# Moving two small tensors and dropping an unused one in a fused attention and MoE kernel

## The reference

```python
# attention (linear, with decay w and bonus u); r, k, v: (4, 8, 768, 48)
for t in range(S):
    cur = einsum('bhd,bhe->bhde', u * k[t], v[t])
    y[t] = einsum('bhd,bhde->bhe', r[t], state + cur)
    state = w * state + einsum('bhd,bhe->bhde', k[t], v[t])
x = y as (3072 tokens, 384)
# first layer, d_ff = 768
h = maximum(maximum(x @ w1, x @ w2), x @ w3);  x = h @ w_out
# second layer, d_ff = 1536
xn = x / sqrt(mean(x * x) + 1e-6) * rms_g
out = (silu(xn @ w_gate) * (xn @ w_val)) @ w_out
```

## Time and profile before

| | |
|---|---|
| median of 3 runs | 918.44 us (918.18 to 918.67) |
| the profiled execution | 918.18 us |
| its span | 916.3 us |
| TensorE matmuls busy | 878.3 us (96%) |
| VectorE, ScalarE, GpSimd busy | 428.6, 318.6, 157.2 us |
| mean granted TensorE clock | 0.989 |

### The profile page before, as it was taken

The page is one execution under the profiler, slowest core; times in us unless marked ns, Lnnn a source line. Parts: engine busy times, 40 slices in busy tenths (PEclk is TensorE's granted clock), DMA queues, the critical chain, the costliest instruction groups (busy, mean ns, idle before and its releaser), DMA issues.

```text
span 916.3 us, 13898 instructions
## 1 busy us (share of the span) xinstructions
PE 878.3 (96%) x4776; PEld 796.2 (87%) x4776; DVE 428.6 (47%) x985; ACT 318.6 (35%) x716; POOL 157.2 (17%) x197
## 2 busy tenths in 40 slices
PE   3689999999999999999989999999999999999998
PEld 3579999999999999999978888888888888888886
DVE  7977565546555564653552342252252342243221
ACT  2453333434333333433443532323233233233212
POOL 5542223232222333200323400000000000000000
PEclk9879999999999999999999999999999999999999
DMA  7263213121311311102222100000000000000000
GB/s 241 92 217 111 60 56 112 61 62 55 112 58 54 115 55 61 55 4 71 76 64 69 35 1 35 1 1 35 1 0 35 0 0 34 0 0 22 13 0 35
DMA packets 45142, 48.28 MB, mean 53 GB/s; under 512 B 3504, under 2 KB 36656, under 8 KB 45104
## 3 DMA queue, kind: packets, MB, share of 16 engines
q1 hardware_dynamic: 45104, 47.79, 16.4%
HBM read 41.88 MB, written 4.72 MB: 51 GB/s over the span
## 4 chain that ended last, share of the span: by engine, by line
PE 90%; DVE 6%; issue 2%; ACT 1%; DMA 0%; DVEq 0%; ACTq 0%
PE h_b L417 16%; PE h_b L419 15%; PE h_b L418 15%; PE y_b L417 8%; PE y_b L419 8%; PE y_b L418 8%; PE a_b L403 4%; PE s_b L388 4%; PE s_b L419 3%; PE s_b L418 3%; PE s_b L417 3%; PE a_b L407 2%; DVE kd L784 2%; PE a_b L411 1%; DVE xl L818 1%
## 5 line engine op out<-in xcount | busy, mean ns | idle before, releaser
L417 PE MATMUL h_b<-xh,Wh 128*128 128x384 f32 (+1 forms) x594 | 216.6, 365 | 5.4 <-DVE xl L818 4.1
L419 PE MATMUL h_b<-xh,Wl 128*128 128x384 f32 (+1 forms) x594 | 208.4, 351 | 0.0
L418 PE MATMUL h_b<-xl,Wh 128*128 128x384 f32 (+1 forms) x594 | 208.3, 351 | 0.0
L417 PE MATMUL y_b<-hh,Wh 128*128 128x512 f32 (+1 forms) x360 | 132.2, 367 | 0.2 <-DVE hl L993 0.2
L419 PE MATMUL y_b<-hh,Wl 128*128 128x512 f32 (+1 forms) x360 | 132.2, 367 | 0.0
L418 PE MATMUL y_b<-hl,Wh 128*128 128x512 f32 (+1 forms) x360 | 132.1, 367 | 0.0
L417 PEld LDWEIGHTS h_b<-xh,Wh 128*128 128x128 f32 x594 | 112.1, 189 | 13.2 <-issue 4.4
L418 PEld LDWEIGHTS h_b<-xl,Wh 128*128 128x128 f32 x594 | 112.3, 189 | 6.4
L419 PEld LDWEIGHTS h_b<-xh,Wl 128*128 128x128 f32 x594 | 111.9, 188 | 6.3
L720 ACT CAST hh<-hB 128x512 fp32r<-128x512 f32 x72 | 44.7, 621 | 163.0 <-DVE hB L988 160.9
L330 POOL TENSOR_TENSOR rd<-rbuf,PR 112x128 f32<-112x128 f32 x96 | 46.0, 481 | 270.0 <-PE a_b L411 236.5
(11 more groups left out here) (124 smaller groups left out, 1334.6 us busy)
## 6 DMA issues: line engine op xcount, KB each, us to landing
vbuf<-in_v SPq DMA_DIRECT2D x24, 320.0 KB, 4.0
kbuf<-in_kT SPq DMA_DIRECT2D x24, 256.0 KB, 3.5
rbuf<-in_rT SPq DMA_DIRECT2D x24, 256.0 KB, 3.7
rnbuf<-in_r SPq DMA_DIRECT2D x24, 192.0 KB, 2.4
knbuf<-in_k SPq DMA_DIRECT2D x24, 192.0 KB, 2.5
x<-in_wA SPq DMA_DIRECT2D x6, 768.0 KB, 7.0
out_t<-xraw SPq DMA_DIRECT2D x5, 768.0 KB, 3.7
wst<-in_gv SPq DMA_DIRECT2D x6, 384.0 KB, 3.1
```

The source lines that it names most:

```text
L417: nc.tensor.matmul(bank[:, 0:n], hi, xhi, start=first, stop=False)
L418: nc.tensor.matmul(bank[:, 0:n], hi, xlo, start=False, stop=False)
L419: return nc.tensor.matmul(bank[:, 0:n], lo, xhi, start=False, stop=last)
```

## The change

The declarations of gcol and eps go from the front to behind onesr, which is the last tensor before the attention group. The unused tensor gap is removed. Nothing else is changed: no instruction, no order, no semaphore.

```diff
-        gcol = sb(ctx, "gcol", [P, KC])
-        eps = sb(ctx, "eps", [P, 1])
-
-        sb(ctx, "gap", [P, 80])
         Wh = sb(ctx, "Wh", [P, F1 * W1F], F32R)
         Wl = sb(ctx, "Wl", [P, F1 * W1F], F32R)
         x2 = sb(ctx, "x2", [P, KC, TOK])
...
         hB = sb(ctx, "hB", [P, 2, GT2])
         xraw = sb(ctx, "xraw", [P, KC, GT2])
         onesr = sb(ctx, "onesr", [P, P], F32R)
+        gcol = sb(ctx, "gcol", [P, KC])
+        eps = sb(ctx, "eps", [P, 1])
```

## The result

The changed kernel took 925.12 us (median of 6 runs, 924.24 to 926.20), the kernel before 918.56 us (6 runs, 917.93 to 920.18). The ratio is 1.0068, with a 95% interval of 1.0055 to 1.0082. I had forecast no change, 918.4 us in a range of 917.0 to 920.5. It is slower, and outside the range.

What follows compares the result with a forecast made beforehand. TensorE was taken to bound the kernel, so only longer matmul-to-matmul times or the first 57 us or so could move the end. All six steps were taken as 0, giving 918.4 us, range 917.0 to 920.5.

Steps and rivals of the forecast that it cites:

- Step 1: TensorE matmuls: operand places off 512-byte multiples cost 0, judged from fp32 matmuls in an attention slot; bounds -9.2 to +9.2 us.
- Rival (a): All 3672 fp32r matmuls: rows starting inside a 512-byte block touch one more, 2.5 ns each, 9.2 us, 927.6 us; chance 0.09.
- Steps 2 to 4 and 6: VectorE, GpSimd, ScalarE operations, and gcol and eps as operands read from another place: each taken as 0.
- Step 5: DMA landings: 0, since later loads are hidden; upper bound 0.2 us on the last store.
- rival (c): DMA writes off a multiple take 23% longer, delaying knbuf pieces around 48 to 52 us: +2.0 us, 920.4; chance 0.03.
- the prediction's estimate: Last stores reading xraw at 128 past: 68 beats for 64 by the skill's DMA page, 6% or 0.12 us.
- Rival (d): Unaligned A, T, kn slow matmuls around 84 attention slots; aligning them gives -1.7 us, 916.7; chance 0.06.
- Rival (b): Early part: shifted timing moves the half-speed clock stretch (36.9 to 57.4 us), +2 us or -2.2 us; chance 0.03 either side.
- my 0.2%: Whole kernel: about 0.2% (1.84 us) is what a measurement can tell from no change.

Runs made afterwards that it cites:

- all64: Kernel before with the unused gap 64 bytes longer, so everything behind it lies 64 bytes higher; 918.91 us against 919.79, ratio 0.9994.
- tail: Changed kernel with gcol and eps declared last, behind ssl and 352 unused bytes, so the large tensors keep their relative places; 919.16 us against 919.54, ratio 0.9995.
- tidy: Kernel before with cur and the small attention tensors behind the large ones, so kn, A, T, PR, PK, PKn start on 512-byte multiples; 919.98 us against 919.54.
- weights64: Kernel before with 64 unused bytes ahead of Xh and again behind Xl, so Xh and Xl lie 64 higher; 924.74 us, ratio 1.0060.
- after_pad: Changed kernel with 64 unused bytes behind eps, putting Xh and Xl at 256 and moving operands at 128; 924.02 us, ratio 1.0048 to the kernel before.
- moving64: Kernel before with 64 unused bytes ahead of xh0 and behind xl1: xh, xl 64 higher, all declared behind them 128 higher; 928.94 us, ratio 1.0108.
- weights128: Kernel before with 128 unused bytes ahead of Xh, moving Xh, Xl and what follows; 923.49 us, ratio 1.0039.
- weights256: Kernel before with 256 unused bytes ahead of Xh, moving Xh, Xl and what follows; 918.72 us, ratio 0.9994.
- high64: Kernel before with 64 unused bytes ahead of Xh and again ahead of Xl: Xh 64, Xl and what follows 128 higher; 922.48 us, ratio 1.0032.
- W64: Kernel before with gap 192 bytes shorter and 192 added behind Wl, so only Wh and Wl lie 192 lower; 930.33 us against 918.75, ratio 1.0128.
- weights32: Kernel before with 32 unused bytes ahead of Xh and 96-byte pad [P, 24] behind Xl, so Xh and Xl lie 32 higher; 924.22 us, ratio 1.0054.

## Why the prediction was wrong

**The view of what bounds the kernel** was right: TensorE through the second layer, and any change of the time had to come from the distance between two matmuls or from the first 57 us.

**Step 1 failed**, in its question and in its row. I asked whether an operand pays for standing off a 512-byte multiple, and the answer to that is no (all64, tail). What counts is how the weights stand to the moving operand, modulo 256 bytes. My working had the number in it, "the two blocks move against each other by 64 bytes only", and then put this term at nothing without a reason. The rows that I tested step 1 on could not show the effect either: they were fp32 matmuls around a slot, kd and rd stood alike, and tidy shows that placing A, kn and T differently changes nothing that can be measured. That no row had an fp32r operand at another place, which I wrote down, should have kept the bound of this step, 9.2 us either way, in the range; the measured cost lies inside it. The size in place of 0 is 0.88 us for six blocks: 6.5 ns for each of the 18 matmuls of a block with Xh and Xl and 3.1 for each of the 9 output matmuls behind them. 36 such blocks are 5.3 us.

**Rival (a)** named the right place, fp32r matmuls that take longer by a fixed amount, and the right side, but the wrong cause and reach: 648 matmuls and their followers pay, not 3672, and the price of 2.5 ns is 6.5. By its condition ("decides from 0.5 ns on over 3672", 1.84 us in all) it did decide.

**Steps 2 to 4 and 6** held: 692 and 621 ns, and rnbuf<-rnbuf,urow at 1003 ns for 1011, with urow at another place again; tail shows gcol and eps to cost nothing. **Step 5** was nearly right. Its row for a write said nothing of the place: urow landed after 4.4 us for 4.3 in the changed kernel, but after 3.5 us in weights64, where it stands at 96 as in the kernel before; so the 23% of rival (c) was the scatter of this one DMA. tail, with every DMA target of the large tensors off 256 bytes, is as fast as before within 0.14%. What did change are the stores that read xraw. The last three, which end the kernel, take 2.1 us in the changed kernel for 2.0:

```profile
out_t<-xraw SPq DMA_DIRECT2D x3, 256.0 KB, 2.1
```

With one more digit the median landing of the three is 2.09 to 2.11 us in the five runs with xraw off a 256-byte multiple (after, after_pad, all64, tail, moving64) and 2.01 to 2.03 in the nine with it on one: some 0.08 us, where the prediction's estimate was 0.12. The five large stores show it as well, 3.76 for 3.65 us, hidden behind matmuls. **Rival (d)** fell with tidy. **Rival (b)**, the clock, moves single runs: profiled kernels with the second layer's 36.72 us start their first x_low between 52.27 us (before) and 53.4 (all64), with different stretches at 1.2 GHz, and weights128 at 53.84 with the early layout of the kernel before. It is no effect of the change, but it is nearly as large as my 0.2%.

**What is left over.** 5.3 us from the second layer, 0.9 from the first and 0.1 from the last stores make 6.3 of the 6.56 us between the medians; the rest is inside the spread of either kernel (2.0 and 2.3 us).

**Shown and not shown.** Shown is that the cost hangs on the difference of the two places modulo 256 and not on either place: the same weights64 and after, the same weights128 and after_pad, and all64, tail and weights256 free. Shown too is that it doesn't fall on the misplaced matmuls alone. That the two reads, of the moving operand and of the next weights, meet in the memory is the simplest reading of it, with the overlap in the timeline behind it, but it is argued. The Trainium skill, "SBUF — State Buffer", section "A bandwidth-pool intuition that's wrong (but worth ruling out)", gives TensorE a second, independent read port for weight loads. It says nothing of places, but a reader would take from it that the two reads don't disturb each other; if this reading of the cost is right, the measured 6.7 ns a matmul stand against that. Open is why 384 columns pay a seventh or less, why two differences in turn (high64) pay less than either, why weights 64 below the moving operand pay less than weights 64 above it (2.8 for 6.1 ns in moving64, one run), and why output matmuls whose operands stand alike lose a part.

## What to carry to other kernels

When tensors are laid out by hand, keep all operands of TensorE at the same place modulo 256 bytes, above all the weights against the moving operand they meet; whether they stand on a round address made no difference to TensorE here. An added or removed tensor of a few bytes between two groups of operands is a change to every matmul that uses both, and their count times the number for their size and difference is a first estimate of its cost. A pad meant to move one tensor moves all that is declared behind it, so work out every place before you read such an experiment. And where a term has no row of its own in the trace, take the nearest row's bound into the range, however well another operation behaves.

## What the runs showed of the hardware

A 512-column fp32r matmul takes 226.7 ns from start to start when its operands stand alike modulo 256 bytes, and 233.3 when the weights stand 64 bytes above the moving operand (W64). The means over the second layer, by how far the weights stand above the moving operand (gate and value matmuls):

| difference | run | ns from start to start | six blocks with Xh and Xl, us |
|---|---|---|---|
| 0 | before | 226.8 | 36.72 |
| 32 | weights32 | 233.0 | 37.47 |
| 64 | weights64, after | 233.2 | 37.60 |
| 128 | weights128, after_pad | 232.7 | 37.43 |
| 192 | moving64, blocks with Wh and Wl | 229.5 | - |
| 256 | weights256 | 226.7 | 36.72 |

Output matmuls with equal places stand 229.8 ns apart in the blocks of weights64 whose gate and value matmuls are misplaced, and 226.7 in the others. At 384 columns a difference of 64 costs about 0.9 ns (0.37 us by 432, W64). Stores from an SBUF tensor 64 or 128 bytes off a 256-byte multiple land 0.08 us later in 2.02 (256 KB) and 0.11 later in 3.65 (768 KB). And in the first 60 us, kernels with the same work ran through one to three stretches at 1.2 GHz, in different places.
